# Routing logits of every second token tile summed on VectorE instead of turned and multiplied on TensorE

## The reference

```python
g = x @ w_gate; silu = g * (1.0 / (1.0 + np.exp(-g)))
x1 = silu * (x @ w_val) @ w_out               # 1536 tokens x 512
do_compute = x1 @ w_skip > 0
logits = x1 @ w_gate_moe2                      # 512 x 8
e_idx = np.argmax(logits, axis=1)              # one expert a token
gate_w = softmax(logits)[e_idx]
y = gate_w * (relu(x1 @ w1[e]) @ w2[e]);  out = x1 + y where do_compute, else x1
```

## Time and profile before

| what | value |
|---|---|
| device time, median of 3 runs | 577.96 us (577.61 to 578.16) |
| the profiled execution | 577.41 us, of which its span 575.5 us |
| granted TensorE clock over the span | 0.979 |
| PE busy | 543.8 us (95%) |
| DVE, ACT, POOL busy | 240.1, 180.9, 95.7 us |
| the stage of x1, by the trace | from about 285 to 406 us |

### The profile page before, as it was taken

One profiled execution on the slowest core, in us unless ns is written; L12 is line 12 of the kernel. 1 busy time (PEld: TensorE's weight loads), 2 busy tenths in 40 slices (PEclk: granted clock), 3 DMA queues, 4 the chain that ended last, 5 costly groups with the idle time before them and its releaser, 6 DMA issues.

```text
span 575.5 us, 10559 instructions
## 1 busy us (share of the span) xinstructions
PE 543.8 (95%) x3752; PEld 460.0 (80%) x3752; DVE 240.1 (42%) x671; ACT 180.9 (31%) x419; POOL 95.7 (17%) x136
## 2 busy tenths in 40 slices
PE   7899999999999999999999999999099999999994
PEld 5677777888888888888888888887089998999993
DVE  5777762333323323322424345542534144255311
ACT  4677862111111111110314335322213133244110
POOL 2234457101111110000000101010101101111111
PEclk9999999999999999999999999999579999999998
DMA  7888532110111111000081114551545787845111
GB/s 214 227 273 249 167 99 75 58 52 10 48 55 55 55 55 55 0 0 1 0 310 56 38 73 167 218 200 73 200 168 183 263 331 282 312 165 189 67 38 37
DMA packets 29510, 73.57 MB, mean 128 GB/s; under 512 B 2816, under 2 KB 15104, under 8 KB 25376
## 3 DMA queue, kind: packets, MB, share of 16 engines
q1 hardware_dynamic: 26592, 63.61, 32.2%
q0 software_dynamic: 2880, 9.47, 4.8%
HBM read 61.77 MB, written 11.29 MB: 127 GB/s over the span
## 4 chain that ended last, share of the span: by engine, by line
PE 86%; DMA 6%; DVE 3%; issue 2%; ACT 1%; POOL 0%; POOLq 0%; DVEq 0%; SPq 0%
PE bank L1237 11%; PE bank L1241 11%; PE bank L1239 11%; PE bank L1406 10%; PE bank L1314 6%; PE bank L1318 6%; PE bank L1316 6%; PE bank L1223 4%; PE bank L1200 3%; PE bank L1418 3%; PE bank L1420 3%; PE bank L1419 3%; PE bank L1179 2%; DMA w_raw<-w 2%; DMA xg<-expert_rows 2%
## 5 line engine op out<-in xcount | busy, mean ns | idle before, releaser
L1237 PE MATMUL bank<-x_hi,w_hi 128*128 128x512 f32 x288 | 112.2, 390 | 0.4 <-issue 0.4
L1241 PE MATMUL bank<-x_hi,w_lo 128*128 128x512 f32 x288 | 112.1, 389 | 0.0
L1239 PE MATMUL bank<-x_lo,w_hi 128*128 128x512 f32 x288 | 112.0, 389 | 0.0
L1406 PEld LDWEIGHTS bank<-xgT,w_sb 128*128 128x128 f32 x704 | 82.8, 197 | 1.9 <-issue 1.2
L1406 PE MATMUL bank<-xgT,w_sb 128*128 128x128 f32 x704 | 83.0, 280 | 0.8 <-ACT xgT L767 0.8
L963 DVE TENSOR_TENSOR sig<-sig,bank 128x512 f32<-128x512 f32 x36 | 24.8, 688 | 127.4 <-ACT sig L680 127.4
L680 ACT ACTIVATE sig<-bank 128x512 f32<-128x512 f32 x36 | 21.5, 598 | 159.6 <-PE bank L1241 159.6
L1237 PEld LDWEIGHTS bank<-x_hi,w_hi 128*128 128x128 f32 x288 | 54.0, 188 | 11.8 <-issue 0.8
L1241 PEld LDWEIGHTS bank<-x_hi,w_lo 128*128 128x128 f32 x288 | 54.1, 188 | 11.3
L1239 PEld LDWEIGHTS bank<-x_lo,w_hi 128*128 128x128 f32 x288 | 54.1, 188 | 11.3
L1314 PE MATMUL bank<-wo_hi,hh_hi 128*128 128x512 f32 x132 | 53.6, 406 | 0.0
(11 more groups left out here) (148 smaller groups left out, 717.9 us busy)
## 6 DMA issues: line engine op xcount, KB each, us to landing
w_raw<-w SPq DMA_DIRECT2D x16, 1024.0 KB, 7.3
w_sb<-w SPq DMA_DIRECT2D x16, 1024.0 KB, 6.3
w_raw<-w_gv SPq DMA_DIRECT2D x12, 512.0 KB, 3.6
va_sb<-v_long SPq DMA_DIRECT2D x10, 512.0 KB, 3.6
xg<-expert_rows POOLq DMA_DIRECT2D x13, 257.0 KB, 2.9
vb_sb<-v_tail SPq DMA_DIRECT2D x10, 320.0 KB, 4.5
q_sb<-qT SPq DMA_DIRECT2D x12, 256.0 KB, 5.0
k_sb<-kT SPq DMA_DIRECT2D x12, 256.0 KB, 6.1
```

The source lines that it names most:

```text
L1237: nc.tensor.matmul(ps[:, :], w_hi[:, u, a, k, :], x_hi[:, k, tok], start=(k == 0), stop=False)
L1239: nc.tensor.matmul(ps[:, :], w_hi[:, u, a, k, :], x_lo[:, k, tok], start=False, stop=False)
L1241: last = nc.tensor.matmul(ps[:, :], w_lo[:, u, a, k, :], x_hi[:, k, tok], start=False, stop=(k == KD - 1))
L1406: last = nc.tensor.matmul(ps, w1_sb[u][:, k, fc], xgT[:, k * P:k * P + P], start=(k == 0), stop=(k == KD - 1))
```

## The change

For tiles with an even number the logits no longer come from TensorE. A new table `w_cols` holds the nine weight columns (eight experts and the skip score) as rows of 512, and two DMAs copy them to all 128 partitions: `route_cols` (16 KB a partition) and `skip_col` (2 KB). VectorE then makes nine multiply-and-sum instructions over x1[t] and one row each (`sum_logits`). Even tiles aren't turned on TensorE nor copied on ScalarE; odd ones stay as they were. The new table lies where `w2_raw` was, `w2_raw` where the first expert's w1 was, and the w1 buffers move on, so the SP queue loads w1 of experts 0, 1 and 2 one step later: after the stores of tiles 6, 7 and 10 instead of at the stage's start and after tiles 6 and 7. The last tiles of TensorE's order are written as the loop body, where before the logits of tile 10 stood three steps ahead of the end.

```diff
@@ homes @@
-        w1_sb = [place(... for i, home in enumerate(((3, 0), (0, 16), (0, 32), (0, 48)))]
-        w2_raw = place("w2_raw", (P, PIECES, FT2 // 2, DM), 3, 16)
+        w1_sb = [place(... for i, home in enumerate(((0, 16), (0, 32), (0, 48), (3, 16)))]
+        w2_raw = place("w2_raw", (P, PIECES, FT2 // 2, DM), 3, 0)
+        route_cols = place("route_cols", (P, E, DM), 3, 16)
+        skip_col = place("skip_col", (P, DM), 1, 46.03125)
@@ SP @@
             sp.wait_ge(h_ready, SLICES + FREE_GV)
-            sp.wait_ge(wo_made, FT1)
+            sp.dma_start(skip_col, w_cols[:, E * DM:].broadcast_to([P, DM])).then_inc(cols_in, 16)
+            sp.dma_start(route_cols.rearrange("p e c -> p (e c)"), w_cols[:, 0:E * DM].broadcast_to([P, E * DM])
+                         ).then_inc(cols_in, 16)
+
+            sp.wait_ge(rows_in_psum, 1)
             load_w2(0)
-            sp.wait_ge(rows_in_psum, 1)
-            load_w1(0)
...
                 if t == NT // 2:
                     sp.wait_ge(h_split, 2 * 6)
-                    load_w1(1)
+                    load_w1(0)
                 if t == NT // 2 + 1:
                     sp.wait_ge(h_split, 2 * 8)
-                    load_w1(2)
+                    load_w1(1)
                 if t == NT // 2 + 2:
                     load_w2(1)
+                if t == NT - 2:
+                    sp.wait_ge(h_split, 2 * 11)
+                    load_w1(2)
@@ VectorE @@
+            def sum_logits(t, u, nth):
+                d.wait_ge(cols_in, 32)
+                d.wait_ge(x1_ready, t + 1 + FREE_OUT)
+                for e in range(E + 1):
+                    if e >= 2:
+                        d.wait_ge(logits_summed, nth * (E + 1) + e - 1)
+                    nc.vector.tensor_tensor_reduce(
+                        out=unread[e % 2], in0=x1[:, u, 0:DM], in1=route_cols[:, e, :] if e < E else skip_col, scale=1.0,
+                        scalar=0.0, op0=ALU.mult, op1=ALU.add, accum_out=logit_sb[:, e:e + 1]).then_inc(logits_summed, 1)
+                d.wait_ge(logits_summed, nth * (E + 1) + E + 1)
...
-                d.wait_ge(logits_in_psum, t + 1)
+                if u:
+                    d.wait_ge(logits_in_psum, nth + 1)
+                    logits = logit_ps
+                else:
+                    sum_logits(t, u, nth)
+                    logits = logit_sb
@@ TensorE @@
-            def tile_of_x1(t, u, first=False):
+            def tile_of_x1(t, u, j, first=False):
                 rows_of_x1(t, u, 0)
-                columns_of_x1(t - 1, 1 - u)
+                if u == 0:
+                    columns_of_x1(t - 1, j - 1)
                 if not first:
                     ranks(t - 2, u)
                 rows_of_x1(t, u, 1)
-                logits_of_x1(t - 1)
+                if u == 0:
+                    logits_of_x1(t - 1, j - 1)
...
-            rows_of_x1(NT - 1, 1, 1, range(FT1 // 2, FT1 - 3))
-            logits_of_x1(NT - 2)
-            rows_of_x1(NT - 1, 1, 1, range(FT1 - 3, FT1))
             ranks(NT - 2, 0)
-            columns_of_x1(NT - 1, 1)
-            logits_of_x1(NT - 1)
+            columns_of_x1(NT - 1, NT // 2 - 1)
+            logits_of_x1(NT - 1, NT // 2 - 1)
             ranks(NT - 1, 1)
```

More of the change, by code:

```diff
@@ L100, in evacuated, with build @@
     return engine, sum(on_act(*u) == engine for u in USES[:use + 1])
-def build(nc, qT, kT, v, va, vb, sizes, w_gv, w_out, w_route, w1, w2, out):
+def build(nc, qT, kT, v, va, vb, sizes, w_gv, w_out, w_route, w_cols, w1, w2, out):
     ctx = ExitStack()
@@ L148, in build @@
         x1 = place("x1", (P, 2, ROW), 1, 24)
-        x1T = place("x1T", (P, DM), 1, 28.125)
+        x1T = place("x1T", (P, DM), 1, 28.03125)
         xg = place("xg", (P, ROW), 1, 0)
@@ L166, in build @@
         first_hi, first_lo = place("first_hi", (P, FT1, P), 3, 0, F32R), place("first_lo", (P, FT1, P), 3, 6, F32R)
-        w1_sb = [place(f"w1_sb{i}", (P, KD, F2), *home) for i, home in enumerate(((3, 0), (0, 16), (0, 32), (0, 48)))]
-        w2_raw = place("w2_raw", (P, PIECES, FT2 // 2, DM), 3, 16)
-        w2_hi = [place(f"w2_hi{u}", (P, FT2, DM), *home, F32R) for u, home in enumerate(((1, 30.25), (2, 0)))]
+        w1_sb = [place(f"w1_sb{i}", (P, KD, F2), *home) for i, home in enumerate(((0, 16), (0, 32), (0, 48), (3, 16)))]
+        w2_raw = place("w2_raw", (P, PIECES, FT2 // 2, DM), 3, 0)
+        route_cols = place("route_cols", (P, E, DM), 3, 16)
+        skip_col = place("skip_col", (P, DM), 1, 46.03125)
+        w2_hi = [place(f"w2_hi{u}", (P, FT2, DM), *home, F32R) for u, home in enumerate(((1, 30.03125), (2, 0)))]
         w2_lo = [place(f"w2_lo{u}", (P, FT2, DM), *home, F32R) for u, home in enumerate(((0, 0), (2, 16)))]
         wr_sb = sb("wr_sb", [P, KD, E + 1])
+        logit_sb = sb("logit_sb", [P, E + 1])
         sums = sb("sums", [P, 2, H])
@@ L287, in build @@
         x1T_ready = sem("x1T_ready")
+        cols_in = sem("cols_in")
+        logits_summed = sem("logits_summed")
         logits_in_psum = sem("logits_in_psum")
@@ L754, in _ @@
                     exp_logits(t - 2, t % 2)
-                copy_columns(t - 1)
+                if t % 2 == 0:
+                    copy_columns(t // 2 - 1)
                 if t - NT // 2 < PIECES:
@@ L1000, in step @@
                     d.wait_ge(choose_step, t * 4 + next(n))
-                d.wait_ge(logits_in_psum, t + 1)
-                nc.vector.tensor_scalar(computes[:, :], logit_ps[:, E:E + 1], 0.0, None, ALU.is_gt)
-                step(nc.vector.tensor_reduce(best[:, :], logit_ps[:, 0:E], AX.X, ALU.max))
-                nc.vector.tensor_scalar(below[:, u, :], logit_ps[:, 0:E], best[:, 0:1], None, ALU.subtract
+                if u:
[4 more added lines that the diff above has]
+                    logits = logit_sb
+                nc.vector.tensor_scalar(computes[:, :], logits[:, E:E + 1], 0.0, None, ALU.is_gt)
+                step(nc.vector.tensor_reduce(best[:, :], logits[:, 0:E], AX.X, ALU.max))
+                nc.vector.tensor_scalar(below[:, u, :], logits[:, 0:E], best[:, 0:1], None, ALU.subtract
                                         ).then_inc(below_ready, 1)
@@ L1055, in _ @@
             split_h(2, 0)
-            choose(0, 0)
+            choose(0, 0, 0)
             with d.Fori(1, NT // 4) as j:
@@ L1354, in tile_of_x1 @@
                 rows_of_x1(t, u, 1)
-                logits_of_x1(t - 1)
+                if u == 0:
+                    logits_of_x1(t - 1, j - 1)
             for q in range(2):
                 rows_of_x1(0, 0, q, hi=first_hi, lo=first_lo)
-            tile_of_x1(1, 1, first=True)
-            with pe.Fori(1, NT // 2 - 1) as j:
-                tile_of_x1(j * 2, 0)
-                tile_of_x1(j * 2 + 1, 1)
-            tile_of_x1(NT - 2, 0)
-            rows_of_x1(NT - 1, 1, 0)
-            columns_of_x1(NT - 2, 0)
-            ranks(NT - 3, 1)
-            rows_of_x1(NT - 1, 1, 1, range(FT1 // 2, FT1 - 3))
-            logits_of_x1(NT - 2)
-            rows_of_x1(NT - 1, 1, 1, range(FT1 - 3, FT1))
+            tile_of_x1(1, 1, 0, first=True)
+            with pe.Fori(1, NT // 2) as j:
+                tile_of_x1(j * 2, 0, j)
+                tile_of_x1(j * 2 + 1, 1, 1)
             ranks(NT - 2, 0)
-            columns_of_x1(NT - 1, 1)
-            logits_of_x1(NT - 1)
+            columns_of_x1(NT - 1, NT // 2 - 1)
+            logits_of_x1(NT - 1, NT // 2 - 1)
             ranks(NT - 1, 1)
```

29 lines of the change are left out of this document (15 added, 14 removed).

## The result

The changed kernel takes **585.32 us** (median of 4 runs, 584.76 to 585.81) against 577.79 us of the kernel before on the same chip (4 runs, 577.25 to 578.16): a ratio of **1.0131, 95% interval 1.0113 to 1.0148**, so 7.5 us slower. The prediction was 578.1, with a range up to 584.0. It missed.

What follows compares the result with a forecast made beforehand. TensorE was taken to set the pace in the x1 stage, 9.7 us a tile. Terms: -8.2 + 3.9 + 3.1 = -1.2, then +0.3, +0.4, +0.65 = +0.15 on 577.96: 578.1 us, range 575.3 to 584.

Steps and rivals of the forecast that it cites:

- the experts' stage as long as before: Sign of a right forecast: the experts' stage, after the x1 stage, keeps its length.
- What is removed: x1 stage, TensorE: transposes (0.46) and logits (0.91) of six even tiles go, 6 x 1.37 = 8.2 us.
- the stalls: x1 stage: TensorE waits for ranks of tiles 4, 6, 8 and transposes of tile 9, 3.9 us in all.
- the walk: Tile-by-tile pass through the changed orders of the x1 stage with profiled durations, giving its stalls.
- The sums at 0.61: VectorE, x1 stage: sums of 512 elements start 0.61 us apart, nine take 5.5, or 5.66 with the last's end.
- the first rival: VectorE's sums slower than 0.61 us: 0.69 adds 3.1 and 0.77 adds 7.1, 581 to 585 us; chance 0.15.
- The end, 3.1 given back: End of x1 stage: ranks of tile 10 wait 3.83 us for VectorE, less some 0.7 already waited: 3.1 us.
- The loads. ... Nothing.: Table lands at about 295 us, before its need at 297.4; moved w1 loads delay nobody: no cost.
- The clock, +0.4: End of x1 stage: the 3.8 us wait may lower the clock for tile 11: 0 to +1.4, taken +0.4 us.
- The scatter clash, 0.5 a scatter: GpSimd's odd-tile scatters clash with the sums reading SBUF: 0.5 us each, +0.65 in all.
- the rival of a longer hold: Scatter held off for more than one instruction: 2 us each gives 582.3, about 4 us gives 590; chance 0.10.
- Sum for the routing alone: All priced terms, confined to the x1 stage: -1.2 + 0.3 + 0.4 + 0.65 = +0.15 us.

Runs made afterwards that it cites:

- e1: Kernel before with SBUF areas 2 and 3 moved 64 bytes on, nothing else changed; ratio 1.0082 (1.0055 to 1.0108).
- e18: The same kernel as e5, run again for a second trace; ratio 1.0041 (1.0021 to 1.0061).
- e5: Changed kernel with areas at their old places, skip_col in dead attention buffers, all discarded products to PSUM; ratio 1.0060 (1.0040 to 1.0081).
- e3: Kernel before with SBUF areas 1, 2 and 3 all moved 64 bytes on; ratio 1.0004 (0.9989 to 1.0020).
- e15: Kernel before with SBUF area 3 alone moved 256 bytes on; 578.39 us, one run.
- e16: Kernel before with SBUF area 3 alone moved 512 bytes on; 577.40 us, one run.
- e2: Changed kernel with areas 2 and 3 another 64 bytes on, 128 in all; ratio to the kernel before 1.0104 (1.0077 to 1.0131).
- e4: Kernel before with SBUF area 3 alone moved 64 bytes on; ratio 1.0075 (1.0050 to 1.0101).
- e6: e5 with tile 10's logits back on TensorE, sums for tiles 0, 2, 4, 6 and 8; ratio to the kernel before 1.0066 (1.0043 to 1.0088).
- e9: e6 with the load of expert 2's w1 behind the store of tile 11; ratio to the kernel before 1.0016 (0.9998 to 1.0034).
- e14: e9 with the load of expert 2's w1 behind all scatters; ratio to the kernel before 1.0010 (0.9992 to 1.0028).
- e13: e5 with sums for tiles 0, 2 and 4 only, expert 2's w1 loaded behind all scatters; 576.81 us, ratio to the kernel before 0.9979.

## Why the prediction was wrong, by its own steps

- **"the experts' stage as long as before", and no word of the h stage.** This is the step that failed. The sum starts from the profiled execution and adds only what the change does in its own stage; the `area` line was in the diff and was not priced. It costs 5.8 us in the h stage, of the 8.2 us between the spans; by the times of e1 it is 4.7 (3.2 to 6.2) of 7.5. With the 2.4 to 3.5 of e18 and e5 that makes 7.1 to 8.2, so the two together account for the 7.5. The experts are 0.9 us longer; whether the placement does that is open, since from the last row number to the end it takes 169.0 to 170.1 us in the traces of before, e3, e5, e15, e16 and e18, all with the operands' distances of before, and 169.8 to 170.7 in the changed kernel, e1, e2 and e4. No rival covered the placement.
- **What is removed (8.2) and the stalls (3.9), so TensorE's last product 4.3 earlier.** Measured 3.0 in the changed kernel, with its areas moved and 1.3 of low clock, and 3.8 in e5 (its last product starts at 395.27, 110.95 us behind the first, where it was 114.72). The wait for x1 of tile 9, 2.62 in the walk, was 1.9 to 3.1. With the clock at full speed this walk was right to about half a microsecond. (The 107 us that it reads as twelve tiles hold eleven; its 9.7 a tile is right.)
- **The sums at 0.61.** 0.61 to 0.62 apart, each 0.69 long; nine 5.63. Right, and the first rival fell. Every second product to PSUM was rightly priced at nothing; every one to PSUM is not free (0.65 apart in e5). The DRAIN section of the Trainium skill's VectorE: DVE Perf Modes says that the next operation does not start before the pipeline is empty, and also that one that is not held starts earlier; the starts at 304.15 and 304.77, of instructions 0.69 long, show the second.
- **The end, 3.1 given back.** 3.7 in the changed kernel, 5.2 in e5, where the clock is at its lower level for the transposes and logits of tile 11, in the changed kernel for the logits alone. But the mechanism was only half of it. e6 took the wait for the sums away and gained nothing, as the copy of x1 of tile 11 stood behind the scatter of tile 9 and this behind the load.
- **"The loads. ... Nothing."** Wrong in two places. The table took 9.6 us, not 6.9 for the pair, and VectorE waited 6.5 us for it. How much of that comes from 128 partitions reading the same rows is not shown: w2's 2 MB, issued at 300.29 in the changed kernel and only behind this load, shared its last 3.9 us. The choice of tile 0 was still in time for its ranks, so this cost nothing. The load of expert 2's w1 at tile 10 was the other half of the end: 2.9 us from e6 to e9. And a load there is not harmless by its distance to the experts, but by what small DMA starts behind it.
- **The clock, +0.4.** Mis-sized, and at the wrong place. I had it at the end alone, where it costs 0.8 in the changed kernel (logits of tile 11 1.88 us, 1.06 before); the wait in the middle of the stage brings 1.3 (changed kernel) to 2.5 (e18) more.
- **The scatter clash, 0.5 a scatter.** Scatters of odd tiles last 1.30 us in place of 0.96 (1.30 at 401.42 above), so 0.34. The mechanism was right and the rival of a longer hold fell. The Trainium skill's SBUF — State Buffer ("Who interferes with whom") has a VectorE instruction with two SBUF inputs contend with a GpSimd one that reads SBUF; the trace agrees (1.30 against 0.96).
- **Sum for the routing alone.** Forecast +0.15, measured +3.5 (2.3 to 4.7) and +2.4 (1.2 to 3.5), with the slower sums of e5 in it. Beside these, the sum took the full clock and a free DMA for granted; what both lack has the same sign. How the rest divides among the three is not shown.

What stays open: which hardware makes the distance of the operands count; whether the placement costs anything in the experts; and why e14, whose trace is as good as e13's, is 2 us slower in its median.

## What to carry to other kernels

Price each line of a diff against every stage that it can reach: a buffer's address is shared by all stages, and 64 bytes here cost 5.8 us in a stage that the sum leaves out, where the best version of the edit gained about 1. When the busiest engine is relieved, look for the next loop by its buffers (here copy to copy into the same buffer), and leave out the added work once to see how much of the gain that loop takes. A bulk load has a price where a small DMA behind it holds a buffer; put it where no such DMA is waited for, and not so late that its user waits.
